# A fused attention, token-mixing and gated-convolution kernel: its last stage run one unit deeper, with a new order on three engines and moved buffers

## The reference

```python
attn = softmax(window of 128 and 4 sinks)(q k^T / 8) v        # stage 1
theta = x @ w_theta
u1 = x + w_tok_r @ (x*cos(theta)) + w_tok_i @ (x*sin(theta))  # stage 2: u1 goes to DRAM
m = u1 + max(u1 @ w_ch, 0)                                    # stage 3 from here
gate_pre[s] = sum over k < 5 of conv_w[k] * m[s - 4 + k]      # causal, depthwise, 5 taps
out = (sigmoid(gate_pre) * (m @ w_val)) @ w_out
```

## The kernel before, in words

| engine | body of unit n before |
|---|---|
| PE | for k: values(n,k), turn(n+2,k); channels(n+1) all; outputs(n) |
| ACT | for k: hi_g(n,k), evac_u(n+2,k); hi_m(n+1) all; evac_out(n); gates(n+1) |
| DVE | gated(n) all; relu_add(n+1) all; conv_rows(n+1) all |
| POOL | lo_g(n) all; lo_u(n+2) all; lo_m(n+1) all |

## Time and profile before

### The profile page before, as it was taken

How to read it: one execution, slowest core, us unless ns; L and a number is a source line. 1 busy time by engine, 2 the same in 40 slices (tenths; PEclk the granted TensorE clock), 3 DMA queues, 4 the chain that set the end, 5 groups by cost and what they waited for, 6 DMA issues and landing times. The chain is left out here.

```text
span 769.9 us, 13823 instructions
## 1 busy us (share of the span) xinstructions
PE 715.6 (93%) x3936; PEld 627.0 (81%) x3936; DVE 439.2 (57%) x1056; ACT 308.5 (40%) x831; POOL 200.0 (26%) x205
## 2 busy tenths in 40 slices
PE   3999999999984799999999999996679999999997
PEld 2998888888973688888888888885679999999995
DVE  3677777777762654564465466451747636654770
ACT  2666666666641422232213322232344244334331
POOL 2111111111110312212212221212743463355221
PEclk9999999999996999999999999997979999999999
DMA  5345445454503100050051006046102012200111
GB/s 162 106 142 163 142 139 164 123 157 128 183 26 116 42 14 15 32 186 27 0 163 68 14 10 209 14 131 225 41 2 83 28 54 82 82 14 27 42 42 41
DMA packets 43328, 66.18 MB, mean 86 GB/s; under 512 B 4000, under 2 KB 20640, under 8 KB 43168
## 3 DMA queue, kind: packets, MB, share of 16 engines
q1 hardware_dynamic: 43296, 65.79, 26.5%
HBM read 46.90 MB, written 18.87 MB: 85 GB/s over the span
## 5 line engine op out<-in xcount | busy, mean ns | idle before, releaser
L232 ACT ACTIVATE probs<-masked,neg_max 128x260 f32<-128x260 f32 (+1 forms) x192 | 93.6, 488 | 82.1 <-DVE neg_max L281 81.7
L351 PE MATMUL ps_s<-k_sb,q_sb 128*128 128x260 f32 (+2 forms) x384 | 108.0, 379 | 12.1 <-DMA k_sb<-kT 12.1
L801 POOL TENSOR_TENSOR z_lo<-z_raw,z_hi 128x512 fp32r<-128x512 f32 x48 | 61.4, 1301 | 211.5 <-ACT z_hi L835 211.5
L964 PE MATMUL acc<-z_hi,w2h 128*128 128x512 f32 x288 | 114.1, 396 | 0.0
L964 PE MATMUL acc<-z_hi,w2l 128*128 128x512 f32 x288 | 112.3, 390 | 0.0
L964 PE MATMUL acc<-z_lo,w2h 128*128 128x512 f32 x288 | 112.2, 389 | 0.0
L216 POOL TENSOR_TENSOR w2l<-x_nat,w2h 128x352 f32 x32 | 29.9, 933 | 184.8 <-DVE w2h L312 184.8
L1241 DVE SCALAR_TENSOR_TENSOR taps<-m_raw,conv_w,taps 128x384 f32<-128x384 f32 x128 | 76.2, 664 | 0.0
L867 DVE TENSOR_TENSOR xT_lo<-ps_x,xT_hi 128x512 fp32r<-128x512 f32 x24 | 16.6, 690 | 98.0 <-ACT xT_hi L822 98.0
L351 PEld LDWEIGHTS ps_s<-k_sb,q_sb 128*128 128x128 f32 x384 | 59.2, 194 | 14.0 <-POOL mask L210 12.1
L398 PE MATMUL ps_o<-v_sb,probsT 128*128 128x64 f32 x384 | 63.8, 261 | 0.0
(11 more groups left out here) (97 smaller groups left out, 1544.0 us busy)
## 6 DMA issues: line engine op xcount, KB each, us to landing
k_sb<-kT SPq DMA_DIRECT2D x16, 390.0 KB, 3.6
q_sb<-qT SPq DMA_DIRECT2D x32, 192.0 KB, 3.2
v_sb<-vP SPq DMA_DIRECT2D x16, 384.0 KB
x_scratch<-x_sb SPq DMA_DIRECT2D x16, 384.0 KB, 3.1
x_nat<-x_scratch SPq DMA_DIRECT2D x24, 256.0 KB, 3.4
x_res<-x_scratch SPq DMA_DIRECT2D x24, 256.0 KB, 4.0
u_scratch<-u_sb SPq DMA_DIRECT2D x24, 256.0 KB, 2.9
u_nat<-u_scratch SPq DMA_DIRECT2D x8, 768.0 KB, 4.6
```

The lines of the kernel that those rows point to most:

```text
L232: nc.scalar.activation(probs[c % 2][:, i, lo:hi], masked[i % 3][:, lo:hi], ACT.Exp, bias=neg_max[:, c, i:i + 1], scale=-1.0, accum_out=row ...
L351: nc.tensor.matmul(ps_s[i % 3][:, lo:hi], q_sb[s][c % 2][:, i * P:(i + 1) * P], k_sb[s][:, first:first + hi - lo], start=True, stop=True). ...
L801: nc.gpsimd.tensor_tensor(z_lo[s % ZR][:, part, :], z_raw[:, part, :], z_hi[s % ZR][:, part, :].bitcast(F32), ALU.subtract).then_inc(z_lo_ ...
L964: last = nc.tensor.matmul(acc[t][:], l, r, start=s == 0 and m == 0 and a == 0, stop=s == T - 1 and m == 1 and a == 2)
```

## The change

Four edits. **Depth**: channels is done for unit n+2 and turn, evac_u and lo_u for n+3; before the loop PE also does channels(1) and turn(2). The loop covers units 0 to 3, then the bodies of the last two batches stand unrolled. **Order of DVE**: the taps of unit n+1 stand between the g products of unit n and the relu_add of unit n+2. **Order of ACT**: gates(n+1) stands ahead of evac_out(n). **Buffers**: a pad of 352 elements behind ident, and conv_w and m_raw moved behind the others; the branch for other sinks and windows, which isn't run with these inputs, gives up one tile for that room.

| engine | body of unit n after |
|---|---|
| PE | for k: values(n,k), turn(n+3,k); channels(n+2) all; outputs(n) |
| ACT | for k: hi_g(n,k), evac_u(n+3,k); hi_m(n+1) all; gates(n+1); evac_out(n) |
| DVE | for k: gated(n,k), then taps 0-2, 3-5, 6-8, 9-10 of n+1; for k: relu_add(n+2,k), then taps 11-12, 13-14, 15-16, 17-19 of n+1 |
| POOL | lo_g(n) all; lo_u(n+3) all; lo_m(n+1) all |

```diff
+ROW_PAD = 352
@@ mix_channels: buffers
-        conv_w = sb("conv_w", [P, CB, TAPS])
-        m_raw = [sb(f"m_raw{r}", [P, CB, HALO + L]) for r in range(2)]
...
         o_sb = [sb(f"o_sb{r}", [P, C]) for r in range(UT)]
+        m_raw = [sb(f"m_raw{r}", [P, CB, HALO + L]) for r in range(2)]
+        conv_w = sb("conv_w", [P, CB, TAPS])
@@ loop
-            with eng.Fori(0, B - 1) as b:
-                body(b, False)
-            body(B - 1, True)
+            with eng.Fori(0, B - 2) as b:
+                body(b, B)
+            body(B - 2, 2)
+            body(B - 1, 1)
+        def ahead(b, c, k, left):
+            j = c + k
+            b2, c2 = (b + j // 2 if j >= 2 else b), j % 2
+            return (b2, c2) if j < 2 * left else None
@@ POOL
-                    if (n := ahead(b, c, 2, last)):
+                    if (n := ahead(b, c, 3, left)):
                         lo_u(*n)
...
             lo_u(0, 0)
+            lo_u(0, 1)
             lo_m(0, 0)
-            lo_u(0, 1)
+            lo_u(1, 0)
@@ ACT
-                    evac_out(b, c)
                     if nxt:
                         gates(*nxt)
+                    evac_out(b, c)
...
+            for k in range(CB):
+                evac_u(1, 0, k)
             act.wait_ge(w_in, 16)
@@ DVE
+            def body(b, left):
+                for c in range(2):
+                    nxt, nxt2 = ahead(b, c, 1, left), ahead(b, c, 2, left)
+                    if nxt:
+                        halo_rows(*nxt)
+                    for k in range(CB):
+                        gated(b, c, k)
+                        if nxt:
+                            conv_rows(*nxt, 3 * k, 3 * k + 3 if k < CB - 1 else 3 * k + 2)
+                    for k in range(CB):
+                        if nxt2:
+                            relu_add(*nxt2, k)
+                        if nxt:
+                            conv_rows(*nxt, 11 + 2 * k, 13 + 2 * k if k < CB - 1 else CB * TAPS)
...
+            for k in range(CB):
+                relu_add(0, 0, k)
+            halo_rows(0, 0)
+            for k in range(CB):
+                conv_rows(0, 0, 2 * k, 2 * k + 2)
+                relu_add(0, 1, k)
+            conv_rows(0, 0, 2 * CB, CB * TAPS)
@@ PE
-                        if nxt2:
-                            turn(*nxt2, k)
-                    if (n := ahead(b, c, 1, last)):
+                        if nxt3:
+                            turn(*nxt3, k)
+                    if (n := ahead(b, c, 2, left)):
                         for k in range(CB):
                             channels(*n, k)
...
+            for k in range(CB):
+                channels(0, 1, k)
+                turn(1, 0, k)
@@ program
+        ctx.enter_context(nc.sbuf_tensor("row_pad", [P, ROW_PAD], F32))
```

More of the change, by code:

```diff
@@ L584, in _ @@
             for i in range(T):
-                link(nc.vector.tensor_scalar(scaled[:], rel[:], float(i * P), None, ALU.add))
-                link(nc.vector.tensor_scalar(upper[:], scaled[:], limit[:, 1:2], None, ALU.is_lt))
-                link(nc.vector.scalar_tensor_tensor(out=masked[:], in0=scaled[:], scalar=0.0, in1=upper[:],
+                shifted = drop[:, i, :]
+                link(nc.vector.tensor_scalar(shifted, rel[:], float(i * P), None, ALU.add))
+                link(nc.vector.tensor_scalar(upper[:], shifted, limit[:, 1:2], None, ALU.is_lt))
+                link(nc.vector.scalar_tensor_tensor(out=masked[:], in0=shifted, scalar=0.0, in1=upper[:],
                                                     op0=ALU.is_ge, op1=ALU.mult))
@@ L598, in body @@
                         dve.wait_ge(scores, g + 1)
-                        nc.vector.scalar_tensor_tensor(out=scaled[:], in0=ps_s[:, 0:S], scalar=SCALE,
+                        nc.vector.scalar_tensor_tensor(out=masked[:], in0=ps_s[:, 0:S], scalar=SCALE,
                                                        in1=keep[:, i, :], op0=ALU.mult,
@@ L1085, in _ @@
             load_u(1, 0)
+            load_u(1, 1)
             def body(b, loads):
                 for c in range(2):
-                    if c < loads:
-                        load_u(b + 1 + c, 1 - c)
+                    if loads:
+                        load_u(b + 2, c)
                     for j in range(UT):
@@ L1186, in evac_out, with body @@
                     nc.scalar.copy(o_sb[j][:], ps_o[(UT * c + j) % 2][:]).then_inc(o_evac, 1)
-            def body(b, last):
+            def body(b, left):
                 for c in range(2):
-                    nxt, nxt2 = ahead(b, c, 1, last), ahead(b, c, 2, last)
+                    nxt, nxt3 = ahead(b, c, 1, left), ahead(b, c, 3, left)
                     for k in range(CB):
                         hi_g(b, c, k)
-                        if nxt2:
-                            evac_u(*nxt2, k)
+                        if nxt3:
+                            evac_u(*nxt3, k)
                     if nxt:
@@ L1214, in _, with relu_add, halo_rows @@
         def _(dve):
-            def relu_add(b, c):
+            def relu_add(b, c, k):
                 n = 2 * b + c
[L1217 to L1227, removed]
+                dve.wait_ge(mixed, CB * n + k + 1)
+                dve.wait_ge(uT_done, CB * n + k + 1)
+                wait_count(dve, m_lo_done, CB * (n - 1))
+                nc.vector.scalar_tensor_tensor(out=m_raw[c][:, k, HALO:HALO + L], in0=ps_c[k % 2][:, 0:L],
+                                               scalar=0.0, in1=uT[c][:, k, :], op0=ALU.max,
+                                               op1=ALU.add).then_inc(m_done, 1)
+            def halo_rows(b, c):
+                dve.wait_ge(m_done, CB * (2 * b + c) + CB)
                 if c == 1:
@@ L1231, in conv_rows @@
                     dve.wait_ge(halo_done, b + 1)
-                for tap in range(TAPS):
-                    for k in range(CB):
[L1234 to L1258, removed]
+            def conv_rows(b, c, begin, end):
+                n = 2 * b + c
+                for j in range(begin, end):
+                    tap, k = j // CB, j % CB
+                    w = conv_w[:, k, tap:tap + 1]
+                    src = m_raw[c][:, k, tap:tap + L]
+                    if tap == 0:
+                        wait_count(dve, gate_done, CB * n)
+                        nc.vector.tensor_scalar(taps[k][:], src, w, None, ALU.mult).then_inc(tap_done, 1)
+                    else:
+                        dve.wait_ge(tap_done, CB * TAPS * n + CB * (tap - 1) + k + 1)
+                        nc.vector.scalar_tensor_tensor(out=taps[k][:], in0=src, scalar=w, in1=taps[k][:],
+                                                       op0=ALU.mult, op1=ALU.add).then_inc(tap_done, 1)
@@ new lines, in gated, with body @@
+            def gated(b, c, k):
+                n = 2 * b + c
+                dve.wait_ge(val_done, CB * n + k + 1)
+                dve.wait_ge(gate_done, CB * n + k + 1)
+                wait_count(dve, g_lo_done, CB * n)
+                nc.vector.tensor_tensor(g_raw[:, k, :], ps_v[k % 2][:, 0:L], gate[:, k, :],
+                                        ALU.mult).then_inc(g_done, 1)
+            def body(b, left):
+                for c in range(2):
+                    nxt, nxt2 = ahead(b, c, 1, left), ahead(b, c, 2, left)
+                    if nxt:
+                        halo_rows(*nxt)
+                    for k in range(CB):
+                        gated(b, c, k)
[6 more added lines that the diff above has]
+                            conv_rows(*nxt, 11 + 2 * k, 13 + 2 * k if k < CB - 1 else CB * TAPS)
@@ L1314, in outputs, with body @@
                     last.then_inc(out_done, 1)
-            def body(b, last):
+            def body(b, left):
                 for c in range(2):
-                    nxt2 = ahead(b, c, 2, last)
+                    nxt3 = ahead(b, c, 3, left)
                     for k in range(CB):
                         values(b, c, k)
-                        if nxt2:
-                            turn(*nxt2, k)
-                    if (n := ahead(b, c, 1, last)):
+                        if nxt3:
+                            turn(*nxt3, k)
+                    if (n := ahead(b, c, 2, left)):
                         for k in range(CB):
```

15 lines of the change are left out of this document (5 added, 10 removed).

## The result

The kernel after takes 779.62 us (median of 6 runs, 777.68 to 780.98); the kernel before, run beside it, 772.54 (6 runs, 771.61 to 773.66). The ratio is 1.0089 with an interval of 1.0069 to 1.0109: 7.1 us slower. The hand-over is the stretch from the work ahead of the loop to the first values, those of unit 0; every later unit is counted from the start of its values to the start of the next unit's.

What follows compares the result with a forecast made beforehand. PE, busy 93% of the span, was taken to bound the kernel. Hand-over -2.8, units 0 to 4 +5.0, unit 5 +0.3, unit 6 +7.6, buffers -0.6 gave +9.5 on 773.1: 782.6 us, range 769 to 788.

Steps and rivals of the forecast that it cites:

- unit 5: Stage 3, unit 5: no lo_u(n+3) there, channels(7,3) waits 0.3 us for its bank, a loss of 0.3 us.
- The price: Taps beside POOL: each POOL instruction holds a multiply-add by 0.75 us (384 columns), or 1.0 us for w_lo.
- The reading that relu_add isn't held: DVE beside POOL: an instruction with a PSUM input is not held; relu_add takes 0.56 us.
- Part 1: Hand-over: PE resumes values 7.0 us later but has done 9.8 us of work; gain 2.8 us, 1.2 to 4.4.
- Part 2: Units 0 to 4: outputs wait 1.0 us each for a copy behind the sigmoids; loss 5.0 us, bounds 0 and 7.
- Part 3: Unit 6: PE resumes 4.5 us late behind values, then outputs wait for block 2; loss 7.6 us, 5.5 to 8.5.
- Part 4: Buffers: new addresses may shorten the matmul steps of ps_c and ps_o; gain 0.6 us, bounds 0 and 3.1.
- 1 (sigmoids just in time, 775): DVE a microsecond faster per unit, units 0 to 4 lose nothing, matmul rates improve to 2 us: 775; chance 0.17.
- 2 (addresses take the gap out of every matmul, 768): Each stage 2 matmul 0.0127 us shorter, stage 2 gains 14.6 us against 9.5 of loss: 768; chance 0.10.
- 3 (POOL holds nothing, 767): POOL does not hold taps in the new places; hand-over gains 7.6, units 0 to 4 lose nothing: 767; chance 0.05.

Runs made afterwards that it cites:

- experiment 4: Kernel after, with POOL waiting for all 20 taps of unit 0 before making w_lo: 779.70 us, ratio 1.0091 to the kernel before.
- experiment 3: Kernel after, with ACT's output copies put back ahead of the sigmoids: 776.39 us, ratio 1.0052 to the kernel before.
- experiment 5: Kernel after with before's orders on DVE and ACT, so only new depth and buffers: 772.62 us, ratio 0.9998 to the kernel before.
- 6: Kernel after with the old orders of DVE and ACT in unit 6 alone: 776.67 us, ratio 1.0052 to the kernel before.
- experiment 1: Kernel before with the new buffers alone (pad, conv_w and m_raw moved): 768.64 us, ratio 0.9947 to the kernel before.
- 2: Kernel before with conv_w and m_raw moved but without the pad: 770.05 us, ratio 0.9968 to the kernel before.
- 9 to 11: Kernel before with a gap of 32, 96 or 64 bytes behind conv_w: 769.58, 771.43 and 772.66 us in single executions.
- experiment 9: Kernel before with a pad of 32 bytes behind conv_w, tiles behind it 128 bytes on: 769.58 us in a single execution.
- experiment 7: Kernel before with the new buffers, ACT's w_hi copies behind evac_u(0,0) and POOL's w_lo behind lo_u(0,0): 765.33 us, ratio 0.9907.
- experiment 8: Kernel before with new buffers, w_hi and w_lo made early, POOL alternating uT_lo of unit 1 and m_lo of unit 0: 761.42 us, ratio 0.9865.

## Why the prediction was right, and which terms were off

The sign, the range and the mechanism held: forecast +9.5 us and 782.6, measured +7.1 and 779.6. The steps, with stage 3 of the two profiles split at the starts of the units' values:

| term | forecast | measured in the profiles |
|---|---|---|
| hand-over | -2.8 | +7.4 late, 9.8 done: -2.4 |
| units 0 to 4 | +5.0 | +3.7; with the 5 x 0.28 of the buffers taken out, +5.1 |
| unit 5 | +0.3 | -0.3; without the buffers -0.1 |
| unit 6 | +7.6 | +7.2 |
| buffers | -0.6 | -1.7 (in units 0 to 5, counted out above) |
| clock in the last unit | none | -1.7 |
| sum | +9.5 | +6.4 |

The 2.84 us in front of stage 3 make the 9.3 us between the two profiled executions; the medians are 7.1 apart.

**The price.** 0.75 us for 384 columns and 1.0 for w_lo carried most of the sum, and they held. Predicted was that the taps of unit 0 end at 570.0; they ended at 572.9, which is 570.1 when the 2.84 us in front of stage 3 are taken off. Predicted was that the taps of a middle unit end 23.3 us after its values begin; measured 23.4. Experiment 4 measured the 1.0 by itself: 4.07 us for four. The reading that relu_add isn't held rested on a row at 606.14, outside the four of POOL (599.49 to 603.43); the timelines of after bear it out, with 0.54 and 0.55 us beside POOL's uT_lo. The Trainium skill, "SBUF — State Buffer", section "Who interferes with whom", has it that a DVE instruction with two SBUF inputs contends with a GpSimd instruction that reads SBUF, and, of DVE's 2-port modes, that whoever issues first gets the shared pair for the whole instruction. The traces agree with the contention and not with the whole length, if that is carried over to the taps: a pair would step by 0.53 + 0.98 = 1.51 us, and steps by 1.28.

**Part 1** held: channels(1) was to start at 547.1 and started at 547.05 (with the 2.84 us taken off), and PE was to resume 7.0 us later, it was 7.4.

**Part 2** held in its place (a wait inside ps_o for the copy behind four sigmoids), and experiment 3, in which it went away with that order, shows the cause. The size was 1.0 us a unit; the idle times were 0.6 to 0.94, and a unit from 1 to 4 took 0.8 to 1.0 longer than before, or 1.1 to 1.2 longer than in experiment 3 with the same buffers (the idle time is counted from the modelled end of a matmul, so it shows less than the starts do).

**Part 3** held. PE resumed 12.35 us after values(6) began, forecast 12.8; block 2 started at 21.0, forecast 21.5. The wait inside ps_o was 1.34 us and not 3, since a low clock of 3.41 us stood in front of it, which the forecast had said that wait would swallow. Experiments 5 and 6 split the 7.2: 4.5 us come from the orders of DVE and ACT, since with the old ones the unit takes 19.33; the other 2.8, against 16.53, from the depth, which uncovers the way to g_lo whatever the order (4.3 in experiment 5, where the clock fell behind that wait).

**Part 4** is the step whose size failed. I took 0.6 out of 0 to 3.1, because no row showed that an address is the cause. Experiments 1, 2 and 9 to 11 show that it is (for ps_c without a rule): 2.4 us of shorter steps in stage 3 when nothing waits, near the upper bound of 3.1; an estimated 1.7 (6 x 0.28) in units 0 to 5 of the kernel after. The upper bound was right in kind: ps_o did fall to the 0.227 of stage 2 and ps_c to the 0.174 of ps_v (8.34 us for 48); but the step of ps_o fell by 0.0053 us (8.39 to 8.20 for 36) and not by 0.007.

**Not in the sum**: the clock in the last unit. Each profile has the same 2.31 us of waiting there. In before and in experiments 3 to 6 and 9 to 11 a stretch of 3.41 us at granted clock 0.50 follows and the unit takes about 24.0 us; in after and in 1, 2, 7 and 8 it doesn't, and the unit takes 22.4. I found no cause in the order of the work, as experiments 3 and 6 end with the same instructions as after. The cause stays open, and 1.6 us of any difference between two profiles here may be this. How often it comes in the executions without a profile isn't known, so the medians hold an unknown part of it.

**The rivals.** 1 (sigmoids just in time, 775): no, units 0 to 4 lost 5.1; but its matmul rates came, 1.7 us of the 2. 2 (addresses take the gap out of every matmul, 768): no, stage 2 steps by 0.227 us after as before, and no step from one matmul of 512 columns to the next is under 0.224 in any profile here. The rows of stage 2, after:

```profile
299.83 0.39 PE L964 MATMUL acc<-z_hi,w2l 128*128 128x512 f32 x1
...
301.42 0.39 PE L964 MATMUL acc<-z_hi,w2h 128*128 128x512 f32 x1
```

Seven steps in 1.59 us. From the Trainium skill, "TensorE: Matmul & The Clock Gate", section "Wait — 56ns, not 53.3ns?", one estimates 0.2158 us for a warm matmul of 512 columns (512 / 2.4 GHz and 2.5 ns). The traces do not agree. 3 (POOL holds nothing, 767): no, by the pairs above and experiment 4.

**What the parts are worth** by medians: buffers -4.3 us (experiment 1, with the last unit's clock in it), depth +4.0 (5 against 1), the new orders of DVE and ACT together +7.0 (after against 5). Of these the order of the sigmoids accounts for 3.2 (3) and unit 6's orders for 3.0 (6), which overlap in unit 6. These are differences of medians of 4 to 10 executions that spread over 2 to 3 us, so each is good to about a microsecond. That the taps between the products cost PE anything apart from these two places was not seen: with the copies first a middle unit takes 26.28 us, as with the old order of DVE.

## What to carry to other kernels

A pipeline that is run one unit deeper does not remove the uncovered work at its start; it moves cover away from its end, and the unit before the last then shows it (here 4.3 us lost, 1.5 of them by a low clock, for 1.8 won). Before two engines' streams are interleaved, look whether they take turns in the trace: work of POOL that nobody waits for yet, as w_lo here, belongs where DVE is idle. Moving w_lo there won 3.3 us (experiment 7 against 1), and letting POOL alternate 3.9 more, with the loop as it was; together with the buffers that is 11 us, and the new loop won nothing. A gain that ends in a wait, as in experiments 3 and 4, is paid out only up to the next engine that is late, so read the next wait before forecasting the gain.

## What the runs showed of the hardware

**A matmul's step can depend on where the tiles lie in SBUF.** 128 x 512 products with g as the stationary tile step by 0.227 us or by 0.233, and the same kernel switches between the two when 32 bytes are put ahead of g and of the tiles around it (experiment 9). In the placements tried, whole multiples of 128 bytes keep the short step, and 32, 64 and 96 bytes beside them give the long one. Of the 128 x 384 products, those of ps_v keep to 8.32 to 8.35 us for 48 in the last unit of all of these, and those of ps_c take 8.32 to 8.49 (0.173 to 0.177 each), by no rule that five placements show.

**A held instruction is held for less than the other's length.** Beside POOL a multiply-add of 0.53 us steps by 1.28, and POOL's subtraction of 0.98 us by 1.28 as well: 0.53 + 0.98 - 1.28 = 0.23 us of each pair overlap. Beside w_lo of 512 columns the hold is 1.0 us (experiment 4), for an instruction that takes 5.02 / 4 = 1.25 with nothing beside it (experiment 8).
